# First product of the last stage by Strassen's scheme, with weight sums formed on chip and streamed from DRAM

## The chip, the cores and the metric

The program runs on one core of one Trainium2 chip. The metric is the device time of one execution in microseconds, read as the median of repeated executions; lower is better.

## What is computed

Attention with a decay mask on four batches of 576 positions, then a mixture of eight experts with two picks for each token, then an MLP whose activation is h cos h. All inputs are float32. Cut to what matters:

```python
x = attention(q, k, v).reshape(2304, 512)
for e in range(8):
    h = np.maximum(x[mask] @ w1[e], 0.0)
    out[mask] += top2_w[mask, k, None] * (h @ w2[e])
x = out                       # 2304 x 512
h = x @ w_in                  # 512 x 2048: the first product of the last stage
g = h * np.cos(h)
return g @ w_out              # 2048 x 512
```

## The kernel before

Every large product is made of three matmuls: each operand is split into a high part in fp32r, written by ScalarE (ACT), and the rest, written by VectorE (DVE), and high times high, low times high and high times low are summed in PSUM. A stationary tile is always 128x128; the moving tile has as many columns as there are tokens in the block (first products), or 512 columns of the output (second products).

**Attention** (lines 1216 to 1286) makes the tokens' rows and the gate's logits. GpSimd scatters each row into the slots of its two experts in DRAM (`x_slots`).

**Experts.** A unit is 640 slots of one expert, five tiles of 128. TensorE walks the units g in a loop; in a unit, step f (0 to 7) makes `product1(g, f + 1)` (line 1303, 24 matmuls of 320 columns), `product2(g, f)` (line 1321, 15 matmuls of 512), and, for f below 5, `transpose_x(g + 1, f)` (line 1209), which turns tile f of the next unit's rows and waits for its load `gath_in`. Meanwhile the weights of the next unit go through the buffer `raw` (two chunks of 512 KB): ACT writes `w_hi` (`w_high`, line 674), DVE `w_lo` (line 1038). SyncE (SP) issues nearly all transfers, in the order of its program and on one queue: in `unit_loads(g)`, for each f, the rows `gath[f]` (line 429) and the ring's chunk (`load_ring`, line 435); after them eight blocks of zeros into `y_slots` (line 446) in units 1 to 5, and the five `store_rows` of the unit's results (line 442). Each `gath[f]` is loaded in the same unit in which its tile is turned. Here unit 0 is written out, units 1 to 6 are the loop, and unit 7, the last, is written out apart (lines 1397 to 1442); during it ACT and DVE also split the sixteen chunks of the last stage's weights (`w_high_last`, `w_low_last`, lines 755 and 1054) into the buffers `w_hi`, `w_lo`, `w2_hi`, `w2_lo`, where all of them stay.

**Last stage.** Six blocks of 384 tokens (TB). `mlp_step(t, f)` on TensorE (line 1444) makes chunk f of 128 hidden features with 12 matmuls of 384 columns (line 1458), and, three steps later, its part of the second product with 9 matmuls of 512 columns (line 1477) into the PSUM banks 0 to 2. Between them a chunk goes ACT, DVE, DVE, ACT, ACT, DVE, ACT, DVE: `turns` (line 797), whole turns (1165), `angle` (1168), abs (802), sin (804), times h (1173), `g_hi` (809), `g_lo` (1176). GpSimd gathers the two expert rows of each token (line 586), ACT and DVE weigh and add them (731, 1109), TensorE turns them (1394), ACT and DVE split them (737, 1116). Outputs leave through ACT and DVE copies of the banks.

## Time and profile before

| | |
|---|---|
| median of 3 executions | 995.12 us (995.02 to 997.41) |
| the profiled execution | 993.64 us |
| its span | 991.7 us |
| TensorE (PE) busy | 973.3 us, 98% |
| weight loads (PEld) busy | 879.6 us |
| VectorE (DVE) busy | 486.5 us |
| ScalarE (ACT) busy | 425.3 us |
| GpSimd (POOL) busy | 104.1 us |
| moved by DMA | 122.02 MB |
| granted TensorE clock over the span | 0.998 |

A row of a group gives the line, the engine, the operation, what is written from what, the shape and the count, then the busy time, the mean duration of one, and the idle time before them with what ended it. Matmuls are pipelined: the duration of one is longer than the distance from one start to the next, and it is the distance that fills TensorE's time.

### The profile page before, as it was taken

To read this page: it belongs to the slowest core of one execution; us is meant where nothing else is said; L and a number is where in the kernel's file an instruction comes from. 1 tells how busy PE (TensorE), PEld (TensorE's weight loads), DVE (VectorE), ACT (ScalarE), POOL (GpSimd) and SP (SyncE) were. 2 spreads that over 40 slices of the span, in tenths; PEclk is the share of its full clock that TensorE was granted. 3 is DMA by queue.
4 is the path that set the end of the run, shared out by engine and by line. 5 is a ranking of instruction groups with operands and counts; after the bars stand their busy time and mean duration, and the time that the engine had idled before them with its cause. 6 is when DMAs were issued, how large, how long until landed. Compare 5 with 4: busy or idle time off the path is not lost.

```text
span 991.7 us, 17311 instructions
## 1 busy us (share of the span) xinstructions
PE 973.3 (98%) x6108; PEld 879.6 (89%) x6108; DVE 486.5 (49%) x944; ACT 425.3 (43%) x779; POOL 104.1 (10%) x106
## 2 busy tenths in 40 slices
PE   8999899999999999999999989999999999999997
PEld 7989789898989988898989979999999999999996
DVE  4788644333334333433434475555555555555554
ACT  1445334233233332332334465555455554545553
POOL 2276500000000000000000231000000001010000
PEclk9999999999999999999999999999999999999999
DMA  9988444436263542626315641010010101010000
GB/s 363 345 321 302 162 165 154 160 109 212 82 225 114 159 168 97 221 95 196 125 71 175 225 164 43 22 46 30 21 53 21 53 21 42 32 42 21 32 0 33
DMA packets 64359, 122.02 MB, mean 123 GB/s; under 512 B 5696, under 2 KB 31552, under 8 KB 64320
## 3 DMA queue, kind: packets, MB, share of 16 engines
q1 hardware_dynamic: 58080, 101.05, 29.7%
q0 software_dynamic: 6240, 20.45, 6.2%
q8 instruction: 25, 0.41, 0.2%
q14 instruction: 14, 0.11, 0.0%
HBM read 83.73 MB, written 37.75 MB: 122 GB/s over the span
## 4 chain that ended last, share of the span: by engine, by line
PE 86%; DMA 5%; issue 3%; POOL 2%; SPq 2%; DVE 1%; ACT 1%; ACTq 0%; POOLq 0%; DVEq 0%
PE ps L1458 20%; PE ps L1477 20%; PE ps L1303 15%; PE ps L1321 14%; PE ps L1209 2%; DMA gath<-x_slots 2%; PE ps L1339 2%; PE ps L1224 2%; PE ps L1407 2%; PE ps L1351 2%; PE ps L1247 2%; PE ps L1419 2%; DMA y_slots<-y_sb 1%; PE ps L1239 1%; POOL x_slots L540 1%
## 5 line engine op out<-in xcount | busy, mean ns | idle before, releaser
L1303 PE MATMUL ps<-xs,w_hi 128*128 (+1 forms) x784 | 182.9, 312 | 0.0
L1038 DVE TENSOR_TENSOR w_lo<-raw,w_hi 128x1024 fp32r<-128x1024 f32 x48 | 58.8, 1225 | 170.8 <-ACT w_hi L674 170.8
L1303 PEld LDWEIGHTS ps<-xs,w_hi 128*128 128x128 f32 x784 | 133.1, 188 | 0.8
L1458 PE MATMUL ps<-x_hi,w_hi 128*128 (+1 forms) x384 | 130.8, 341 | 0.1
L1458 PE MATMUL ps<-x_hi,w_lo 128*128 (+1 forms) x384 | 129.1, 336 | 0.0
L1458 PE MATMUL ps<-x_lo,w_hi 128*128 (+1 forms) x384 | 129.1, 336 | 0.0
L797 ACT ACTIVATE turns<-ps 128x384 f32<-128x384 f32 x96 | 47.2, 491 | 184.2 <-PE ps L1458 184.2
L1303 PE MATMUL ps<-xs,w_lo 128*128 (+1 forms) x392 | 121.2, 309 | 0.0
L1165 DVE TENSOR_SCALAR turns<-turns 128x384 f32<-128x384 f32 x96 | 37.3, 388 | 168.1 <-ACT turns L797 168.1
L1477 PE MATMUL ps<-w_hi,g_hi 128*128 128x512 f32 x288 | 112.6, 391 | 2.1 <-DVE g_lo L1176 2.1
L1477 PE MATMUL ps<-w_hi,g_lo 128*128 128x512 f32 x288 | 113.3, 393 | 0.0
L1477 PE MATMUL ps<-w_lo,g_hi 128*128 128x512 f32 x288 | 113.3, 393 | 0.0
L674 ACT ACTIVATE w_hi<-raw 128x1024 fp32r<-128x1024 f32 x48 | 50.8, 1059 | 141.3 <-PE ps L1321 107.8
L1321 PE MATMUL ps<-w_hi,hs_lo 128*128 128x512 f32 x245 | 96.2, 393 | 0.0
L1321 PE MATMUL ps<-w_lo,hs_hi 128*128 128x512 f32 x245 | 96.2, 393 | 0.0
L1321 PE MATMUL ps<-w_hi,hs_hi 128*128 128x512 f32 x245 | 95.8, 391 | 0.0
L668 ACT ACTIVATE hs_hi<-ps 128x320 fp32r<-128x320 f32 x98 | 42.3, 437 | 79.3 <-PE ps L1303 79.3
L1458 PEld LDWEIGHTS ps<-x_hi,w_hi 128*128 128x128 f32 x384 | 72.1, 188 | 3.7 <-issue 0.5
L1458 PEld LDWEIGHTS ps<-x_hi,w_lo 128*128 128x128 f32 x384 | 72.1, 188 | 3.1
L1303 PEld LDWEIGHTS ps<-xs,w_lo 128*128 128x128 f32 x392 | 73.7, 188 | 0.8
L1458 PEld LDWEIGHTS ps<-x_lo,w_hi 128*128 128x128 f32 x384 | 72.1, 188 | 0.0
L586 POOL DMA_INDIRECT y<-y_slots,pos_now x42 | 41.8, 995 | 276.3 <-PE ps L1394 266.9
(167 smaller groups left out, 1649.4 us busy)
## 6 DMA issues: line engine op xcount, KB each, us to landing
raw<-weights SPq DMA_DIRECT2D x80, 512.0 KB
y_slots<-zeros_sb SPq DMA_DIRECT2D x42, 256.0 KB, 3.6
gath<-x_slots SPq DMA_DIRECT2D x40, 256.0 KB, 3.5
y_slots<-y_sb SPq DMA_DIRECT2D x40, 256.0 KB, 2.1
qk<-qk SPq DMA_DIRECT2D x18, 512.0 KB
kv<-kv SPq DMA_DIRECT2D x18, 512.0 KB
out<-out_sb SPq DMA_DIRECT2D x18, 256.0 KB, 2.1
x_slots<-zeros_sb SPq DMA_DIRECT2D x8, 256.0 KB, 7.7
```

The source lines that it names most:

```text
L586: nc.gpsimd.indirect_dma_start(out=y[j][:, :], out_offset=None, in_=y_slots, in_offset=bass.IndirectOffsetOnAxis(ap=pos_now[:, k, j:j + 1] ...
L668: nc.scalar.activation(hs_hi[:, par, half * HALF:(half + 1) * HALF], ps[5 + half][:, 0:HALF], ACT.Relu).then_inc(relu_done, 1)
L674: nc.scalar.activation(w_hi[:, f * CHUNK:(f + 1) * CHUNK], raw[:, f % 2, :], ACT.Copy).then_inc(hi_done, 1)
L797: nc.scalar.activation(turns[f % 2][:, :], h_bank(f)[:, 0:TB], ACT.Copy, scale=PER_TURN, bias=ROUND).then_inc(turn_done, 1)
L1038: tt(w_lo[:, at], raw[:, f % 2, :], w_hi[:, at].bitcast(F32), ALU.subtract).then_inc(split_done, 1)
L1165: ts(whole[:, :], whole[:, :], -ROUND, None, ALU.add).then_inc(whole_done, 1)
L1209: last_one = nc.tensor.transpose(x_bank(g, j)[:, k * BLK:(k + 1) * BLK], gath[j][:, k * P:(k + 1) * P], ident)
L1224: last_one = nc.tensor.matmul(ps[half][0:C, n * C:(n + 1) * C], qk_sb[t % 3][rows, 1, n, :], qk_sb[t % 3][rows, 0, n, :], start=True, stop ...
L1303: last_one = nc.tensor.matmul(ps[5 + half][:, 0:HALF], w[:, at:at + P], xs[:, bass.ds(g % 2, 1), a, k, half * HALF:(half + 1) * HALF].rear ...
L1321: last_one = nc.tensor.matmul(ps[j][:, :], a[:, f % 2, j * BLK:(j + 1) * BLK], w[:, at:at + DM], start=f == 0 and i == 0, stop=f == FE - 1 ...
L1458: last_one = nc.tensor.matmul(h_bank(f)[:, 0:TB], w[:, cols], a[:, bass.ds(par, 1), k, :].rearrange("p a s -> p (a s)"), start=k == 0 and ...
L1477: last_one = nc.tensor.matmul(ps[j][:, :], a[f2 % 2][:, rows], w[:, cols], start=f2 == 0 and i == 0, stop=f2 == FT - 1 and i == 2)
```

## The change

**The scheme.** The hidden features are taken in eight pairs of chunks (`FP`), the tokens in four blocks of 384, 640, 640 and 640 (`SIZES`), each in two halves (`HALVES`: 192, 320, 320, 320). A slot is one block and one pair: 32 slots. In a slot the first product is a 2x2 block product (the two halves of the 512 input dimensions, the two chunks of the pair, the two halves of the tokens). It is made of seven products (`strassen(slot, o)`, 6 matmuls each of 192 or 320 columns) in place of eight. Both operands need sums: four of the weights (S), four of the tokens. Each of the seven results is copied or added into `p1_sb`, `u2`, `u3`, `u4` and the four quarters `h_sb` by ACT (one) and DVE (seven operations, `drain`). Only PSUM banks 5 and 6 hold these results (`p_bank`), so product i waits until product i - 2 has been taken away. The second product keeps its tile shape, as steps of 3 matmuls (`second`) for each tile and chunk, put between the seven products of the next slot. `h` is scaled to turns beforehand, through the gates (`gate1` times 1/2pi), which takes away one DVE operation of each chunk; the outputs are scaled back (`TURN`).

**The weights.** ACT and DVE form, for each pair, the high and low parts and the sums in `stage1` and `stage2`, in units 1 to 4 of the experts, two pairs in a unit (`pair_high`, `pair_low`). SP stores each pair into new DRAM tensors `w1_pairs` and `w2_pairs` and reads them back in every slot (`load_w1`, `load_w2`). A pair is 2 x 512 KB read, and 1.835 MB + 1.049 MB stored. The splitting in the last unit falls away. The six-block loop becomes straight code; block 0's tokens are split with the sums in `x_first`, the others in `x_odd` and `x_even`.

```diff
+SIZES = (3, 5, 5, 5)
+HALVES = tuple(n * C // 2 for n in SIZES)
+SLOTS = NBK * FP
+A11, A12, A22, S_FROM, A_W = 0, 256, 512, 768, 1792
+ORDER = ((A11, 0), (A12, 1), (S_FROM + 256, 4), (S_FROM + 512, 5), (A22, 6), (S_FROM, 3), (S_FROM + 768, 2))
+DRAINED = (0, 1, 2, 3, 4, 6, 7)
+PREP_UNITS = FP // 2
```

SP, the pairs' transfers and the streamed weights:

```diff
+            def load_pair(i):
+                if i >= 2:
+                    sp.wait_ge(pair_lo, 4 * (i - 1))
+                for half in range(2):
+                    sp.dma_start(raw_pair[i % 2][:, half, :], weights[E * FE + 2 * i + half]).then_inc(pair_in[i % 2], 16)
+            def store_pair(i):
+                sp.wait_ge(pair_lo, 4 * (i + 1))
+                sp.dma_start(w1_pairs[i].rearrange("p (a n) -> p a n", a=2), stage1[i % 2][:, :, :].bitcast(F32)
+                             ).then_inc(pair_out[i % 2], 16)
+                sp.dma_start(w2_pairs[i].rearrange("p (a n) -> p a n", a=2), stage2[i % 2][:, :, :].bitcast(F32)
+                             ).then_inc(pair_out[i % 2], 16)
+            for i in range(2):
+                load_pair(i)
             for j in range(TPU):
                 store_rows(0, j)
+            def next_pair(i):
+                store_pair(i)
+                if i + 2 < FP:
+                    load_pair(i + 2)
...
                     load_ring(g, f, e_next)
+                    if isinstance(g, int) and g <= PREP_UNITS and f == 4:
+                        next_pair(2 * (g - 1))
...
-            with sp.Fori(1, E - 2) as g:
+            for g in range(1, E - 2):
                 unit_loads(g)
                 for j in range(E):
                     zero_block(E * TPU + j + (g - 1) * E)
                 for j in range(TPU):
                     store_rows(g, j)
+                if g <= PREP_UNITS:
+                    next_pair(2 * (g - 1) + 1)
...
+            def load_w1(slot):
+                if slot >= 2:
+                    sp.wait_ge(p_done, 7 * (slot - 1))
+                sp.dma_start(w1_sb[slot % 2][:, :, :].bitcast(F32), w1_pairs[slot % FP].rearrange("p (a n) -> p a n", a=2)
+                             ).then_inc(w1_in[slot % 2], 16)
```

DVE, the low parts and the sums of the weights (ACT's `pair_high` writes the high parts of the same 1024, 512, 256 and 1024 columns); both stand in step f of unit g behind the splits of w and x:

```diff
+            def pair_low(i, q):
+                src = raw_pair[i % 2]
+                if q == 0:
+                    dve.wait_ge(pair_hi, 4 * i + 1)
+                    tt(stage2[i % 2][:, 1, :].rearrange("p (b n) -> p b n", b=2), src[:, :, DM:CHUNK],
...
+                if q == 2:
+                    a11, a12 = src[:, 0, 0:2 * P], src[:, 0, 2 * P:4 * P]
+                    a21, a22 = src[:, 1, 0:2 * P], src[:, 1, 2 * P:4 * P]
+                    link(tt(sums[:, 0, :], a21, a22, ALU.add))
+                    link(tt(sums[:, 1, :], sums[:, 0, :], a11, ALU.subtract))
+                    link(tt(sums[:, 2, :], a11, a21, ALU.subtract))
+                    tt(sums[:, 3, :], a12, sums[:, 1, :], ALU.subtract).then_inc(pair_sums, 1)
+                if q == 3:
+                    dve.wait_ge(pair_hi, 4 * i + 4)
+                    tt(stage1[i % 2][:, 1, S_FROM:A_W], sums[:, :, :].rearrange("p m n -> p (m n)"),
+                       stage1[i % 2][:, 0, S_FROM:A_W].bitcast(F32), ALU.subtract).then_inc(pair_lo, 1)
...
+                    if isinstance(g, int) and g <= PREP_UNITS:
+                        pair_low(2 * (g - 1) + f // 4, f % 4)
```

DVE, the middle of one slot of the last stage (`reduce`, `product` and `g_low` are its part of the cosine chain; ahead of these lines stand `reduce`, `g_low`, `product`, `drain` and `g_low` for the end of the slot before and for product 1):

```diff
+                reduce(slot, 0)
+                drain(slot, 2, u2, p1_sb)
+                product(slot, 0)
+                g_low(slot, 0)
+                dve.wait_ge(drained, 7 * slot + 2)
+                drain(slot, 3, u3, u2)
+                if p == 0 and b > 1:
+                    rows_out(b - 1, 1)
+                if b + 1 < NBK:
+                    ahead(b, p)
+                dve.wait_ge(drained, 7 * slot + 3)
+                drain(slot, 4, h_sb[1], u3, True)
+                reduce(slot, 1)
+                drain(slot, 5, u4, u2)
+                drain(slot, 5, h_sb[2], u3)
+                product(slot, 1)
+                reduce(slot, 2)
+                g_low(slot, 1)
+                dve.wait_ge(drained, 7 * slot + 5)
+                drain(slot, 6, h_sb[3], u4)
+                product(slot, 2)
...
 PE:
+            def strassen(slot, o):
+                b, i, n = slot // FP, 7 * slot + o, HALVES[slot // FP]
+                w, m = ORDER[o]
+                if o == 0:
+                    pe.wait_ge(w1_in[slot % 2], 16 * (slot // 2 + 1))
+                if slot % FP == 0:
+                    pe.wait_ge(x_lo_done, 7 * b + o + 1)
+                if i >= 2:
+                    before = (i - 2) % 7
+                    if before == 0:
+                        pe.wait_ge(p1_copied, (i - 2) // 7 + 1)
+                    else:
+                        pe.wait_ge(drained, 7 * ((i - 2) // 7) + DRAINED[before])
+                x = x_of(b)
+                for k in range(2):
+                    cols = slice(w + k * P, w + (k + 1) * P)
+                    for j, (hl, a) in enumerate(((0, 0), (1, 0), (0, 1))):
+                        last_one = nc.tensor.matmul(p_bank(i)[:, 0:n], w1_sb[slot % 2][:, hl, cols], x[:, a, m, k, :],
+                                                    start=k == 0 and j == 0, stop=k == 1 and j == 2)
+                last_one.then_inc(p_done, 1)
...
+            BEHIND = {10: (1, 1, 2, 1, 2, 2, 1), 6: (1, 1, 1, 1, 1, 1, 0)}
+            for slot in range(SLOTS):
+                b, p = slot // FP, slot % FP
+                todo = steps_of(slot - 1) if slot > 0 else []
+                at = 0
+                for o in range(7):
+                    strassen(slot, o)
+                    if todo:
+                        for step_ in todo[at:at + BEHIND[len(todo)][o]]:
+                            second(slot - 1, *step_)
+                        at += BEHIND[len(todo)][o]
```

Here `ahead(b, p)` prepares the next block during slot p of block b: for each tile ACT weighs, DVE adds and ACT copies it, and for each block seven highs on ACT, seven lows and four sums on DVE, each twice as wide as a half.

**SP at the end of an expert unit before** (`raw` and `gath` are the ring's chunk and the rows, an ISA row is a count for a wait), from the ring's last chunk on; the loop then turns back to `gath`:

```order
L435 ISA [waits split_done]
L435 DMA raw<-weights 128x1024
L446 ISA
L446 DMA y_slots<-zeros_sb 512x1x128
...
L442 ISA [waits y_act]
L442 DMA y_slots<-y_sb 128x512
```

The same place in the change, between the stores of unit 1 and the loads of unit 2 (`w_pairs` are the new DRAM tensors):

```order
L500 DMA y_slots<-zeros_sb 512x1x128 x8
L496 DMA y_slots<-y_sb 128x512 [waits y_act]
...
L531 DMA w_pairs<-stage_1 128x3584 [waits pair_lo]
L533 DMA w_pairs<-stage_1 128x2048
L527 DMA raw_pair<-weights 128x1024 [waits pair_lo]
L527 DMA raw_pair<-weights 128x1024
L547 TENSOR_LOAD meta
L547 ISA x2
L548 TENSOR_LOAD meta
L548 ISA x2
L483 ISA [waits tx_done]
L483 DMA gath<-x_slots 128x512
```

Four transfers now stand ahead of the first rows and the first ring chunk of the next unit, and SP waits for DVE's last low part of the pair before it issues any of them.

**ACT at the start of the last stage in the change**, between the experts' last result and the first copy out of a Strassen product (`p_sb` is `p1_sb`):

```order
L871 ACTIVATE y_sb<-ps 128x512 [waits y_out1]
L857 ACTIVATE x_first<-first_sums 128x384 [waits x_sums] x3
L857 ACTIVATE x_first<-raw 128x384 [waits xT_copied]
L900 ACTIVATE p_sb<-ps 128x192 [waits p_done]
L907 ACTIVATE turns<-h_sb 128x192 [waits drained]
```

Before, `turns` followed the copy to `y_sb` directly; four copies of tokens and the copy of product 0 now stand between them.

## Rows read from the trace of the kernel before

**Rows 1.** The page, part 1: busy time of each engine, share of the span, instructions.
```profile
PE 973.3 (98%) x6108; PEld 879.6 (89%) x6108; DVE 486.5 (49%) x944; ACT 425.3 (43%) x779; POOL 104.1 (10%) x106
```
**Rows 2.** Windows: stretch, engines' busy time, granted clock, DMA share, GB/s.
```profile
10.00:14.00 4.00, 3.40 (x64) 2.97 (x62) 3.03 (x6) 0.60 (x1) 2.00 (x2) 1.00 1.03 407
22.00:26.00 4.00, 4.00 (x69) 3.64 (x70) 2.66 (x7) 1.14 (x2) 0.80 (x1) 1.00 1.04 397
200.00:560.00 360.00, 357.81 (x2027) 323.80 (x2026) 134.28 (x192) 122.94 (x201) 0.92 (x2) 1.00 0.45 148
576.00:640.00 64.00, 62.52 (x324) 57.07 (x325) 39.23 (x73) 37.68 (x72) 14.39 (x15) 1.00 0.26 83
```
**Rows 3.** Timeline, TensorE, one step of the last stage: start us, us, engine, what.
```profile
762.68 0.33 PE L1458 MATMUL ps<-x_hi,w_hi 128*128 x1
764.79 0.39 PE L1477 MATMUL ps<-w_hi,g_hi 128*128 128x512 f32 x1
766.87 0.60 PE L1394 MATMUL ps<-table_sb,y 128*128 128x128 f32 x4
767.23 0.42 PE L1458 MATMUL ps<-x_hi,w_hi 128*128 x1
```
**Rows 4.** Timeline, first and last matmul of the last stage.
```profile
575.99 0.44 PE L1458 MATMUL ps<-x_hi,w_hi 128*128 128x384 f32 x1
...
986.60 0.39 PE L1477 MATMUL ps<-w_hi,g_lo 128*128 128x512 f32 x1
```
**Rows 5.** Timeline, TensorE, an expert step at a unit's start.
```profile
227.79 0.31 PE L1303 MATMUL ps<-xs,w_hi 128*128 x1
231.30 0.40 PE L1321 MATMUL ps<-w_hi,hs_hi 128*128 128x512 f32 x1
235.47 0.65 PE L1209 MATMUL ps<-table_sb,gath 128*128 128x128 f32 x4 [0.56 <-DMA gath<-x_slots]
```
**Rows 6.** Timeline, TensorE, attention: matmuls of 16 columns, back to back.
```profile
91.73 1.07 PE L1275 MATMUL ps<-wg,xT 128*128 128x16 f32 x8
92.65 0.64 PE L1280 MATMUL ps<-table_sb,xT 128*128 128x128 f32 x4
```
**Rows 7.** Groups of DVE and ACT instructions with their shapes: busy, mean ns, idle.
```profile
L1038 DVE TENSOR_TENSOR w_lo<-raw,w_hi 128x1024 fp32r<-128x1024 f32 x48 | 58.8, 1225 | 170.8 <-ACT w_hi L674 170.8
L1173 DVE TENSOR_TENSOR angle<-ps,angle 128x384 f32<-128x384 f32 x96 | 53.4, 557 | 7.8 <-ACT angle L804 0.5
L1124 DVE SCALAR_TENSOR_TENSOR hs_lo<-ps,hs_hi 128x256 fp32r<-128x256 f32 x7 | 2.9, 419 | 2.7 <-ACT hs_hi L746 2.7
...
L809 ACT ACTIVATE g_hi<-angle 128x384 fp32r<-128x384 f32 x96 | 48.8, 508 | 1.7 <-PE ps L1477 1.7
```
**Rows 8.** Waits: engine, line waited for, total us, times, longest.
```profile
PE ps L1209 <- DMA gath<-x_slots: 6.8, 7, 3.3
```
**Rows 9.** Timeline, SP's issues at the same unit's start.
```profile
226.14 4.07 SPq L442 DMA_DIRECT2D y_slots<-y_sb  x5
232.60 0.36 SPq L429 DMA_DIRECT2D gath<-x_slots  x1
```
**Rows 10.** Timeline, ACT and DVE at the same unit's start.
```profile
229.54 1.05 ACT L674 ACTIVATE w_hi<-raw 128x1024 fp32r<-128x1024 f32 x1
238.05 1.06 ACT L674 ACTIVATE w_hi<-raw 128x1024 fp32r<-128x1024 f32 x1 [6.11 <-DMA raw<-weights]
243.12 1.06 ACT L674 ACTIVATE w_hi<-raw 128x1024 fp32r<-128x1024 f32 x1 [2.88 <-PE ps L1321]
250.51 1.06 ACT L674 ACTIVATE w_hi<-raw 128x1024 fp32r<-128x1024 f32 x1 [3.00 <-PE ps L1321]
...
230.62 1.23 DVE L1038 TENSOR_TENSOR w_lo<-raw,w_hi 128x1024 fp32r<-128x1024 f32 x1 [1.66 <-ACT w_hi L674]
```
**Rows 11.** DMA issues: tensor, issuer, count, KB each, median us to landing.
```profile
y_slots<-y_sb SPq DMA_DIRECT2D x40, 256.0 KB, 2.1
...
wg<-gates_w SPq DMA_DIRECT2D x1, 32.0 KB, 7.7
```

More of the change, by code:

```diff
@@ L300, in logit_bank, with x2_bank @@
             return ps[7 - k % 2]
-        def walk_mlp(eng, step, tail=0):
-            for f in range(FT):
-                step(0, f)
-            with eng.Fori(1, NTB) as t:
-                for f in range(FT):
-                    step(t, f)
-            for f in range(tail):
-                step(NTB, f)
-        PREP_AT = (4, 8, 12)
-        def x2_bank(t, j):
-            return ps[j] if isinstance(t, int) and t == 0 else ps[3]
-        O_BANK = (2, 3)
+        def x2_bank(n):
+            return ps[n] if n < 3 else ps[{4: 3, 5: 4, 7: 3}.get(n, 7)]
@@ L321, in x_bank, with outs @@
+        def outs(b, j, odd_ones):
+            return sum((n + 1) // 2 if not odd_ones else n // 2 for n in SIZES[:b]) + j // 2 + 1
         def x_bank(g, j):
@@ L1185, in _, with drain @@
-            walk_mlp(dve, mlp_step, MLP_LAG + 1)
+            x2_sum(0, 2)
+            x2_sum(0, 3)
+            for at in range(2, 7):
+                x2_low(0, at)
+            def drain(slot, o, to, other, subtract=False):
+                n, i = HALVES[slot // FP], 7 * slot + o
+                dve.wait_ge(p_done, i + 1)
+                p = p_bank(i)[:, 0:n]
+                if subtract:
+                    tt(to[:, 0:n], other[:, 0:n], p, ALU.subtract).then_inc(drained, 1)
+                else:
+                    tt(to[:, 0:n], p, other[:, 0:n], ALU.add).then_inc(drained, 1)
@@ new lines, in g_low, with rows_out @@
+            def g_low(slot, q):
+                n, c = HALVES[slot // FP], 4 * slot + q
+                part, half = QUARTERS[q]
+                cols = slice(half * n, (half + 1) * n)
+                dve.wait_ge(g_hi_done, c + 1)
+                tt(g_lo[:, slot % 2, part, cols], angle[q][:, 0:n], g_hi[:, slot % 2, part, cols].bitcast(F32), ALU.subtract
+                   ).then_inc(g_split, 1)
+            def rows_out(b, j):
+                tile = FIRST_TILE[b] + j
+                dve.wait_ge(m2_done, final_step(b, j))
+                if b == 0 and j == 1:
+                    dve.wait_ge(y_all, 1)
+                above(dve, out_out[tile % 3], 16 * (tile // 3))
+                ts(out_sb[tile % 3][:, :], ps[j][:, :], TURN, None, ALU.mult).then_inc(out_dve, 1)
@@ L1486 @@
+            for step_ in steps_of(SLOTS - 1):
+                second(SLOTS - 1, *step_)
 def kernel(q, k, v, moe_w_gate, moe_w_noise, moe_noise, moe_w1, moe_w2, moe2_w_in, moe2_w_out):
```

676 lines of the change are left out of this document (422 added, 254 removed).

## The prediction

> **What bounds the kernel now.** I read the page first: TensorE is busy for 973.3 of 991.7 us and no other engine for half of that [rows 1]. So only two things can change the time: how long TensorE's instructions fill it, and new waits of TensorE. The windows say where it waits now: 2.2 us in the experts' 360 us, and 1.5 us in the first 64 us of the last stage [rows 2]. The clock is granted in full there, so every length below is one at 2.4 GHz. The timeline gives the true price of a matmul, the distance between starts. A step of the last stage is 2.11 us for 12 matmuls of 384 columns and 2.08 us for 9 of 512, and four transposes add 0.36 us [rows 3]. 96 steps and 15 transposed tiles make 402.2 + 5.4 = 407.6 us; from the first to the last matmul the stage takes 411.0 us [rows 4], so 3.4 us are waits at its ends. In the experts 24 matmuls of 320 columns take 3.51 us, 0.146 each [rows 5].
>
> The waits view has the row that matters most here: TensorE waits for the rows `gath` seven times, 6.8 us in all [rows 8]. Most of it is before unit 1, half a us at each later unit's start. It is small, but it says that the first load of each unit has no slack. In the timeline SP issues it at 232.60, and TensorE starts its transpose at 235.47, 2.87 us after, having waited [rows 5, 9].
>
> **The first product.** A slot of 320 columns fills TensorE for 42 x 0.146 + 30 x 0.231 = 6.13 + 6.93 = 13.06 us; 24 of them 313.4 us. For 192 columns no row exists. From 320 columns down, 0.029 us go with each 64 columns (0.146 at 320, 0.176 at 384), which gives 0.088 us. But eight matmuls of only 16 columns, each with its own 128x128 stationary tile, start 0.115 us apart (91.73 to 92.65) [rows 6]: there is a floor that columns don't lower. I take 0.112, by the row of 16 columns, since a Strassen matmul also changes its stationary tile each time; the ends are 0.088 and 0.115. A slot of 192 columns is then 42 x 0.112 + 18 x 0.231 = 4.70 + 4.16 = 8.86 us, eight of them 70.9 us. With the transposes the stage's filled time is 313.4 + 70.9 + 5.4 = 389.7 us against 407.6: **17.9 us less**. The seven-for-eight saving is there for 320 columns and is turned round for 192: 4.70 us where the same tokens cost 4.22 (two steps) before.
>
> The Trainium skill (TensorE: Matmul & The Clock Gate, "Back-to-back issue gap") gives a warm gap of N/2.4 + 2.5 ns, 82.5 ns for 192 columns; by it block 0 would cost 42 x 0.0825 x 8 = 27.7 us, an estimate, in place of 37.6. The 0.115 us between starts of 16-column matmuls disagree with that rule, and the row decides here; it stays as a rival.
>
> **New waits in the last stage.** DVE and ACT get more work and only two banks hold products. A DVE operation costs 0.419 us at 256 columns, 0.557 at 384, 1.225 at 1024 [rows 7]; between and beyond I take 0.35 at 192, 0.49 at 320, 0.82 at 640. A slot has 19 on DVE: 9.3 us of 13.06 at 320 columns, which fits, and 6.7 of 8.86 at 192.
> - Slot 0: product 2 waits for ACT's copy of product 0, which stands behind the last experts' copy and four copies of tokens (five of about 0.5 us by the 384-column row [rows 7]); the drains on DVE stand behind five low parts of 0.55 us. There is no second product to fill the gaps. I walk it to about 9.3 us for 4.7 of work, and slot 1 to 2 us late: +6.6.
> - Slots 6 and 7: DVE also makes one low and four sums, then five lows, 4.1 us each time, 10.8 us where TensorE needs 8.86: +1.9 twice, and about as much again since the two-bank hand-over leaves DVE no queue to work from. Slots 2 to 5: about +1 each with the tiles' adds. Block 0 in all: **+14**.
> - Opening block 1: the second product of tile 1 waits for DVE's copy of the old bank, which the program puts behind the drain of the next slot's product 1: +3.4.
> - The other slots of 320 columns: +0.2 each for late drains, +4. At the end the last chunk's chain, as before, 2.5.
>
> Together 24; the stage is 389.7 + 24 = 413.7 us against 411.0: **+2.7**. The gain is spent. With only slot 0 and DVE's bound it would be 10 (stage -11), with twice my waits 35 (+14).
>
> Weights: 2.88 MB a slot. Against a rate of 397 to 407 GB/s in the busiest windows [rows 2], 7.2 us of 8.86 in block 0 and of 13.06 later; with two gathered tensors for each tile (0.52 MB, 0.8 us a slot) block 0 just fits, and its slots are longer than that anyway. Cost 0; without that cover, rival B.
>
> **New waits in the experts: what decides.** ACT's added 3.1 us a pair (1024 + 512 + 256 + 1024 columns) and DVE's 5 us lie beside a TensorE that waits for neither. The transfers don't. At a unit's end SP now waits for the pair's last low part: ACT's `w_hi` ends at 230.6, its sums' high part at 231.6, DVE's `w_lo` ends at 231.85 and the low part 1.2 us later, 233.0 [rows 10]. Only then it issues a store of 1.835 MB, one of 1.049 MB, two loads of 0.52 MB, and behind them `gath[0]` and the ring's chunk, on one queue. That this queue is served in order shows in the transfers: 32 KB (`wg`) needed 7.7 us to land in the loaded first stage, 256 KB 2.1 us on an idle queue [rows 11]. At 390 GB/s, a little under the busiest windows since these are mostly stores, 3.93 MB are 10.1 us. `gath[0]` lands at 233.0 + 10.1 + 2.87 = 246.0 and TensorE, in order, stands at its transpose from 235.47: **10.5 us**, at the ends of units 1, 2 and 3. After unit 4 nothing is loaded: 2.88 MB, 7.4 us, 7.8 us late. Sum 39.3. The ring's chunk lands about 2 us after `gath[0]`, and what hangs on it has that slack.
> - The Trainium skill (DMA: Bandwidth & Descriptors, "Where 436 GB/s comes from") says that HBM transfers bind at about 358 GB/s; by it the four waits would be 3.4 us longer in sum, an estimate. The 407 GB/s of a window don't agree.
> - Inside a unit the even pair goes out in step 4, ahead of ring chunk 5. The steps are 7.39 us (243.12 to 250.51 [rows 10]); DVE is done with the pair 4.2 us into the step after 257.9, the backlog ends at 272.2 and the chunk lands near 276.5, wanted at 272.3. The late `w_hi`, and behind it two pair operations, hold back `relu` and `h_low` until about 1.1 us after TensorE wants them: 3 x 1.1 = 3.3 (ends 0 and 4 each).
> - Before unit 1 the first two pairs' loads (2.1 MB, 5.4 us) delay the y stores by about 2 us: 1.5.
>
> Experts: **+44.1**, ends 30 and 55. The last unit loses its splits, which TensorE didn't wait for: 0; its queue carries 6.8 MB (17.5 us) long before the y rows.
>
> **Sum.** 993.6 (the profiled execution) + 2.7 + 44.1 = 1040.4; the median of the runs is 1.5 us above that execution: **1042 us**.
>
> **Rivals.**
> A, faster: the transfers don't queue. If the sixteen rings serve the new transfers beside the old ones, `gath[0]` is only 1 us late at each of four units, the half-unit delay goes, and the stage decides: at its low end 995.1 + 4 + 1.5 - 11 = 989.6. It decides while a unit's wait stays under 1.5 us. Against it stand the 7.7 us of a 32 KB load, and that SP is held until 233.0, 0.4 us behind the old issue, in any case. Chance 0.09.
> B, slower still: the streamed weights or the stage's hand-overs bind. If reads with 2.88 MB a slot reach only 290 GB/s, a slot of block 0 is 11 us, +5, and with twice my stage waits +11: 1058; more with stores slower than 390 GB/s, up to 1070. For it: nothing in this trace stores so much. Chance 0.13.
> C, no floor under 192 columns: matmuls at 0.088 us, the lower end above, make 42 x 0.024 x 8 = 8 us less than my sum, 1034. DVE would bind block 0 at about the same length, so little of it would be seen. Chance 0.05. The Trainium skill's gap rule, named above, is this case.
> The forecast itself: 0.73.
>
> **Numbers.** About 0.3% (3 us) is what a measurement of this kernel tells from no change. A faster result needs A: 0.08; within 0.3% 0.02; slower 0.90. The range takes the experts' and the stage's low ends nearly together (995 + 30 - 7 = 1018) and reaches B's middle (1062); outside are A and B's tail.
>
> **What would show it.** In the changed profile: TensorE's wait for `gath<-x_slots` near 46 us in all with a longest of 10 to 11 us, four times at unit starts; SP's store of w_pairs issued some 3 us after the y stores; 42 matmuls of 320 columns in 6.1 us and of 192 in 4.7; block 0 about 85 us long, later slots 13.1 to 13.5. Right in sign for the wrong reason would be a stage far over 420 us with no long `gath` waits; wrong altogether if those waits stay under 2 us.

## The result, and the profile after

The changed kernel takes 1061.45 us (median of 4, 1058.85 to 1064.73) against 996.12 us for the kernel before on the same chip: 1.0657 times as long, interval 1.0623 to 1.0691. The forecast was 1042 us with 1018 to 1062.

| span of the profiled execution, by stretch | forecast | measured |
|---|---|---|
| up to TensorE's first transpose of unit 1 (176.77 before, 182.35 now) | +1.5 | +5.6 |
| waits for `gath` after units 1 to 4 | +39.3 | +45.2 |
| the rest of the experts (the last stage opens at 634.30, 575.99 before) | +3.3 | +7.5 |
| the last stage, first to last matmul (421.5 us, 411.0 before) | +2.7 | +10.5 |
| behind the last matmul | 0 | -1.4 |
| sum | +46.8 | +67.4 |

The second row is 13.09 + 12.53 + 13.12 + 8.25 less the same waits before, 0.56 [rows 5], 0.32, 0.48 and 0.46 us; the third is what is left of 58.3. The page, its row of engines, which answers to [rows 1], and the granted clock in tenths over 40 slices of the span:

```profile
PE 981.9 (93%) x6288; PEld 878.5 (83%) x6288; DVE 587.5 (55%) x1238; ACT 494.8 (47%) x976; POOL 96.6 (9%) x93
PEclk9999998997998998989999998999999999999999
```

TensorE is busy for 8.6 us more, in a span that is 67.4 us longer: what came is waiting. The waits view (waiter, line, what ended it, us in all, times, longest):

```profile
PE ps L1507 <- DMA gath<-x_slots: 54.2, 6, 13.1
PE ps L1757 <- ACT p_sb L900: 5.5, 10, 1.8
PE ps L1773 <- DVE out_sb L1408: 3.2, 1, 3.2
PE ps L1757 <- DVE h_sb L1378: 3.1, 2, 2.0
PE ps L1619 <- DVE y_sb L1228: 1.9, 1, 1.9
```

The first row answers to the 6.8 us of [rows 8]. The timeline shows one of these waits. SP's issues (start, length, what):

```profile
228.03 7.11 SPq L500 DMA_DIRECT2D y_slots<-zeros_sb  x8
235.25 5.28 SPq L496 DMA_DIRECT2D y_slots<-y_sb  x5
243.47 0.33 SPq L531 DMA_DIRECT2D w_pairs<-stage  x1
243.84 0.43 SPq L533 DMA_DIRECT2D w_pairs<-stage  x1
244.32 2.24 SPq L527 DMA_DIRECT2D raw_pair<-weights  x2
249.19 0.35 SPq L483 DMA_DIRECT2D gath<-x_slots  x1
```

TensorE in the same timeline, with its last matmul ahead of the wait:

```profile
242.69 0.39 PE L1619 MATMUL ps<-w_hi,hs_lo 128*128 128x512 f32 x1
256.17 1.11 PE L1507 MATMUL ps<-table_sb,gath 128*128 128x128 f32 x4 [13.09 <-DMA gath<-x_slots]
```

ACT there, a copy of y, a pair's high part and the first split of the next unit:

```profile
239.50 0.60 ACT L764 ACTIVATE y_sb<-ps 128x512 f32<-128x512 f32 x1 [4.09 <-DMA y_slots<-y_sb]
240.95 1.05 ACT L817 ACTIVATE stage<-sums 128x1024 fp32r<-128x1024 f32 x1
257.35 1.06 ACT L757 ACTIVATE w_hi<-raw 128x1024 fp32r<-128x1024 f32 x1 [14.70 <-DMA raw<-weights]
```

And DVE, a copy of y and the pair's last low part:

```profile
238.78 0.69 DVE L1228 COPY y_sb<-ps 128x512 f32<-128x512 f32 x1 [3.95 <-DMA y_slots<-y_sb]
242.23 1.22 DVE L1298 TENSOR_TENSOR stage<-sums,stage 128x1024 fp32r<-128x1024 f32 x1
```

From the store of the pair (243.47) to the transpose (256.17) it is 12.7 us; the forecast had 13.0. But the store itself is late. The copies of the y rows waited about 4 us for earlier y stores, 1.6 and 1.8 us before. Before, SP had issued the last store of zeros 1.8 us ahead of the first y store; now the ring's last chunks come late, behind the even pair's transfers, and the zeros end at 235.14, directly ahead of the y stores. So the pair's last low part ends at 243.4, when TensorE has just come to rest. The forecast had it 1.9 us ahead of TensorE.

The windows show what had not been in the forecast at all (stretch, busy times, granted clock, DMA share, GB/s):

```profile
243.00:260.00 17.00, 3.92 (x19) 3.84 (x19) 2.81 (x5) 2.52 (x4) 0.00 (x0) 0.60 0.88 339
460.00:475.00 15.00, 6.75 (x29) 6.25 (x29) 2.32 (x3) 1.98 (x3) 0.00 (x0) 0.66 0.87 319
636.00:650.00 14.00, 12.13 (x56) 11.43 (x57) 9.09 (x27) 8.22 (x23) 5.79 (x6) 0.63 0.69 236
745.00:850.00 105.00, 103.30 (x572) 91.44 (x572) 77.95 (x162) 69.87 (x146) 9.38 (x9) 1.00 0.58 223
```

In each long wait of TensorE and behind it, and in the first slots of the last stage, part of the stretch has the lower clock, 1.2 GHz in place of 2.4. Before, it was granted in full there [rows 2]. The four transposes behind the wait take 1.11 us, 0.65 before [rows 5].

The last stage by blocks (634.30 is its first matmul):

```profile
634.30:721.40 87.10, 79.47 (x483) 68.27 (x482) 60.85 (x167) 57.53 (x150) 15.62 (x16) 0.92 0.73 275
721.40:833.20 111.80, 107.43 (x585) 94.78 (x586) 80.04 (x169) 73.51 (x157) 10.24 (x10) 0.98 0.62 238
833.20:942.70 109.50, 107.80 (x597) 95.58 (x597) 81.83 (x170) 74.84 (x158) 4.09 (x4) 1.00 0.61 233
942.70:1055.80 113.10, 112.00 (x607) 99.52 (x606) 75.74 (x165) 70.22 (x151) 0.00 (x0) 1.00 0.52 196
```

Block 0 takes 87.1 us, about 85 in the forecast. In it the chain that ended last runs for long stretches between ACT and DVE alone, here in slot 4 (start, length, what):

```profile
676.55 0.46 ACT angle L915
677.03 0.37 DVE angle L1392
677.42 0.36 ACT g_hi L922
677.79 0.31 ACT angle L913
678.12 0.46 ACT angle L915
...
678.89 0.36 DVE h_sb L1380
679.27 0.37 ACT turns L907
```

### The profile page after: what moved, and what is told of

Read it like the earlier page. It is cut to its first block, busy times and chain, and to the rows that moved or that the text cites. A ratio compares the mean times of both kernels' runs of the same rounds, so it can differ in the third digit from the quotient of the medians.

```text
span 1059.1 us, 17609 instructions
## 1 busy us (share of the span) xinstructions
PE 981.9 (93%) x6288; PEld 878.5 (83%) x6288; DVE 587.5 (55%) x1238; ACT 494.8 (47%) x976; POOL 96.6 (9%) x93
## 4 chain that ended last, share of the span: by engine, by line
PE 59%; ACT 10%; DVE 10%; DMA 8%; SPq 5%; issue 5%; POOL 1%; DVEq 0%; ACTq 0%; POOLq 0%
PE ps L1601 11%; PE ps L1773 11%; PE ps L1619 10%; PE ps L1757 10%; DMA gath<-x_slots 3%; ACT angle L915 3%; DMA raw<-weights 3%; PE ps L1704 2%; ACT angle L913 2%; PE ps L1716 2%; DVE angle L1392 2%; SPq L500 2%; PE ps L1522 2%; DMA y_slots<-y_sb 2%; ACT g_hi L922 2%
## 5 line engine op out<-in xcount | busy, mean ns | idle before, releaser
L1773 PE MATMUL ps<-w_sb,g_hi 128*128 128x512 f32 x576 | 183.6, 400 | 3.2 <-DVE out_sb L1408 3.2
L1757 PE MATMUL ps<-x_odd,w_sb 128*128 128x320 f32 x672 | 118.2, 311 | 2.7 <-ACT p_sb L900 1.4
L1757 PEld LDWEIGHTS ps<-x_odd,w_sb 128*128 128x128 f32 x672 | 106.7, 189 | 14.8 <-issue 3.8
L1773 PE MATMUL ps<-w_sb,g_lo 128*128 128x512 f32 x288 | 113.2, 393 | 0.0
L1773 PEld LDWEIGHTS ps<-w_sb,g_hi 128*128 128x128 f32 x576 | 99.4, 191 | 10.5 <-issue 3.5
L907 ACT ACTIVATE turns<-h_sb 128x320 f32<-128x320 f32 (+1 forms) x128 | 56.4, 441 | 65.9 <-DVE h_sb L1378 55.3
L1392 DVE TENSOR_TENSOR angle<-h_sb,angle 128x320 f32<-128x320 f32 (+1 forms) x128 | 58.7, 458 | 47.9 <-ACT angle L915 45.7
L913 ACT ACTIVATE angle<-angle 128x320 f32<-128x320 f32 (+1 forms) x128 | 57.0, 445 | 36.2 <-DVE angle L1386 36.1
L1399 DVE TENSOR_TENSOR g_lo<-angle,g_hi 128x320 fp32r<-128x320 f32 (+1 forms) x128 | 58.5, 457 | 26.5 <-ACT g_hi L922 19.1
L922 ACT ACTIVATE g_hi<-angle 128x320 fp32r<-128x320 f32 (+1 forms) x128 | 57.0, 445 | 34.0 <-DVE angle L1392 31.5
## 6 DMA issues: line engine op xcount, KB each, us to landing
y_slots<-zeros_sb SPq DMA_DIRECT2D x42, 256.0 KB, 4.0
gath<-x_slots SPq DMA_DIRECT2D x40, 256.0 KB, 3.6
y_slots<-y_sb SPq DMA_DIRECT2D x40, 256.0 KB, 2.1
```

The lines of the kernel that those rows point to most:

```text
L907: nc.scalar.activation(turns[c % 2][:, 0:n], h_sb[q][:, 0:n], ACT.Copy, bias=ROUND).then_inc(turn_done, 1)
L913: nc.scalar.activation(a, a, ACT.Abs).then_inc(abs_done, 1)
L922: nc.scalar.activation(g_hi[:, slot % 2, part, half * n:(half + 1) * n], angle[q][:, 0:n], ACT.Copy).then_inc(g_hi_done, 1)
L1392: tt(angle[q][:, 0:n], h_sb[q][:, 0:n], angle[q][:, 0:n], ALU.mult).then_inc(g_done, 1)
L1399: tt(g_lo[:, slot % 2, part, cols], angle[q][:, 0:n], g_hi[:, slot % 2, part, cols].bitcast(F32), ALU.subtract).then_inc(g_split, 1)
L1757: last_one = nc.tensor.matmul(p_bank(i)[:, 0:n], w1_sb[slot % 2][:, hl, cols], x[:, a, m, k, :], start=k == 0 and j == 0, stop=k == 1 and ...
```

## Experiments on the experts' waits

Two questions: are these waits the place in SP's queue, and nothing of the change's own work on ACT and DVE? And what does the lower clock cost?

**r3_before_bulk**: the kernel before, with bytes alone (loads into a buffer that nothing reads, and SP's loop over the units written out).

```diff
                 for j in range(TPU):
                     store_rows(g, j)
+                for c in range(RING):
+                    sp.dma_start(bulk[:, c * CHUNK:(c + 1) * CHUNK], weights[c]).then_inc(bulk_in, 16)
...
```

> The kernel before, with eight loads of 0.52 MB (4.19 MB in all, into memory that nothing reads) issued by SP behind the y stores at the end of units 1 to 5, and nothing else of the change. Queue theory: SP issues them at about 230.3 on the clock of rows 9, they take 10.7 us at 390 GB/s, gath[0] lands 2.9 us behind them at 243.9, so TensorE waits 8.8 us at each of five unit starts, 44 us in all; the time is about 995 + 42 = 1037, or 1040 to 1045 if the clock is low after each wait. Rival (transfers share the rings, and the added work of ACT and DVE made the waits of the changed kernel): waits under 2 us, time under 1003.

Measured: 1045.60 us (two runs, 1044.21 and 1046.99), 1.0502 times before (1.0479 to 1.0526). SP's issues in its timeline:

```profile
231.80 4.27 SPq L493 DMA_DIRECT2D bulk<-weights  x8
237.49 0.35 SPq L432 DMA_DIRECT2D gath<-x_slots  x1
```

And its waits view:

```profile
PE ps L1215 <- DMA gath<-x_slots: 50.7, 8, 9.8
```

Eight loads of 0.52 MB between the y stores and `gath` make waits of 8.88, 9.79, 8.89, 8.79 and 8.90 us, with no sum of weights formed anywhere. So bulk transfers in that place of the queue are enough, without any work on ACT and DVE.

**r1_gath_ahead**: the odd pair's transfers behind the first `gath` of the next unit, and so in front of its first ring chunk.

```diff
                         load_rows(f, v_next)
+                        if f == 0 and isinstance(g, int) and 1 < g <= PREP_UNITS + 1:
+                            next_pair(2 * (g - 2) + 1)
...
-                if g <= PREP_UNITS:
-                    next_pair(2 * (g - 1) + 1)
```

> The changed kernel with gath[0] of units 2 to 5 issued ahead of the pair's stores and loads; ring chunk 0 stays behind them. Queue theory: TensorE's wait for gath falls from 54 us to under 10 in all, but chunk 0 lands about 14 us after the store is issued, ACT's w_hi holds back relu, and TensorE waits 8 to 10 us for DVE's hs_lo two products later; the time falls only to 1045 to 1055. Rival (the wait belongs to the rows alone, the ring has slack enough): no new wait, the time falls by about 45 to 1015.

Measured: 1051.64 us (two runs, 1049.76 and 1053.51). The wait moved to the next thing behind the transfers, as its waits view shows:

```profile
PE ps L1507 <- DVE xs L1200: 27.7, 4, 7.8
PE ps L1507 <- DMA gath<-x_slots: 11.7, 5, 4.5
```

The second transposes wait for DVE's low part of the tokens, which stands behind the low part of a weight chunk that came late; I had expected the wait two products later. Moving the bulk past one small load gives back 10 of 58 us, since the ring's chunk is as urgent.

**r2_warm**: matmuls of zeros in the waits, 52 after units 1 to 3 and 34 after unit 4 (TensorE's loop over these units is written out).

```diff
+                    if f == 0 and isinstance(g, int) and g > 1:
+                        pe.wait_ge(xs_done, TPU * (g + 1))
+                        for _ in range(52 if g < 5 else 52*2//3):
+                            nc.tensor.matmul(ps[7][:, 0:P], zeros_sb[:, :], zeros_sb[:, :], start=True, stop=True)
```

> The changed kernel with 52 matmuls of zeros (35 at the last) on TensorE ahead of its wait for gath[0] in units 2 to 5, into a bank that the transposes then overwrite; they fill the wait and take away none of it. Clock theory: the half clock that the profile shows from 2 to 3 us into each wait until 3 us behind it comes from the idle time; with it filled the granted clock stays full through these stretches, and the matmuls behind the wait run at full pace: 1.3 to 2 us less for each of four waits, 5 to 8 us in all, 1054. Rival (the clock falls for another reason, or costs nothing there): no change, 1061, or more if the zeros end later than the rows land.

Measured: 1058.08 us (1055.54 to 1061.15), 3.4 us less. Its window over the stretch that had 0.60:

```profile
243.00:260.00 17.00, 15.74 (x130) 15.33 (x129) 2.73 (x5) 2.23 (x6) 0.00 (x0) 1.00 0.89 339
```

The lower clock is gone there, and little comes of it: the two intervals against before overlap (1.0601 to 1.0658 and 1.0623 to 1.0691). It is a price of some 3 us, not of 10. The trace shows where some of the rest went: from the last matmul of a unit to the transposes it is now 48.0 us in sum for 47.0, and inside units 1 and 3 stand two waits of 0.83 and 0.92 us for DVE's `hs_lo` that the changed kernel does not have.

**r4_spread**: the same bytes in pieces, one or two behind each ring chunk (`behind_ring`); a pair's store is cut in three and its load in two, and the stores of zeros move to steps 0, 1, 4 and 5.

```diff
-                if g <= PREP_UNITS:
-                    next_pair(2 * (g - 1) + 1)
+                    if isinstance(g, int):
+                        behind_ring(g, f)
...
```

> The changed kernel with the same bytes moved in the experts, but each pair's store cut in three pieces and each load in two, one or two issued behind each ring chunk, and the zero blocks moved from the end of a unit to its steps 0, 1, 4 and 5. No step of 7.4 us then has over 2.4 MB (6 us). Queue theory: the gath wait falls to under 9 us in all, the half clock goes, and the experts take within 6 us of before; the time is about 1061 - 52 = 1008. Rival (the bytes or the added ACT and DVE work cost it, wherever they are issued): over 1035.

Measured: 1004.00 us (1001.53 to 1004.06). TensorE's waits for `gath` are 6.6 us in all, as before the change, and the last stage opens at 577.7. Nearly the whole of the experts' +58.3 us was the placement.

**p1_pool_queue**: the same transfers, whole, issued by GpSimd on its queue; SP's calls go.

```diff
+            for i in range(FP):
+                pool.wait_ge(pair_lo, 4 * (i + 1))
+                pool.dma_start(w1_pairs[i].rearrange("p (a n) -> p a n", a=2), stage1[i % 2][:, :, :].bitcast(F32)
+                               ).then_inc(pair_out[i % 2], 16)
+                pool.dma_start(w2_pairs[i].rearrange("p (a n) -> p a n", a=2), stage2[i % 2][:, :, :].bitcast(F32)
+                               ).then_inc(pair_out[i % 2], 16)
+                if i + 2 < FP:
+                    load_pair(i + 2)
...
```

> The changed kernel (1061.45 us) with only this moved: the loads and stores of the pairs (raw_pair<-weights, w_pairs<-stage) are issued by GpSimd, whose queue is empty then, instead of by SP. The same bytes at the same times, or a little earlier, since GpSimd waits for nothing but the pair's last low part. Theory (the waits are the order within SP's one queue, not the bytes): gath and the ring's chunks go beside the pairs' packets, TensorE's waits for gath fall from 54.2 us to 7 to 15 and the experts cost 2 to 12 us more than before the change: 1005 to 1016, best guess 1009. Rival (the 16 DMA engines are the limit and share alike, so that 256 KB beside 3.93 MB still land 5 us or more late): 1025 or more.

Measured: 1000.70 us (999.55 to 1001.34), 1.0057 times before (1.0042 to 1.0073); 61 us less than the changed kernel for one move of code, and better than my best guess of 1009. GpSimd's issues in its timeline:

```profile
234.37 0.54 POOL L659 DMA_DIRECT2D w_pairs<-stage  x1 [27.26 <-DVE stage L1290]
234.89 0.54 POOL L661 DMA_DIRECT2D w_pairs<-stage  x1
235.42 1.05 POOL L652 DMA_DIRECT2D raw_pair<-weights  x2
```

SP's first loads of the same unit start:

```profile
233.25 0.36 SPq L483 DMA_DIRECT2D gath<-x_slots  x1
233.88 0.35 SPq L489 DMA_DIRECT2D raw<-weights  x1
234.49 0.33 SPq L483 DMA_DIRECT2D gath<-x_slots  x1
```

TensorE's transpose:

```profile
236.03 0.65 PE L1499 MATMUL ps<-table_sb,gath 128*128 128x128 f32 x4
```

And the window that answers to the third of [rows 2]:

```profile
200.00:560.00 360.00, 360.00 (x2053) 327.52 (x2052) 157.08 (x241) 132.96 (x222) 17.72 (x31) 1.00 0.65 236
```

TensorE has no wait at the transposes at 236.03 with 3.9 MB on their way, and none in the 360 us in which it waited for 2.2 before [rows 2]. Two things changed with this one move, and the rows tell them apart. SP no longer waits for the pair's last low part, so the first rows leave 1.1 us ahead of GpSimd's first store, and the ring's first chunk 0.5 us ahead; at the other three unit ends the rows are 1.5 us ahead. The first rows land after 2.7 us (before, it was 2.87 us from their issue to the transpose [rows 5, 9]). The loads beside the bulk are slow: the second rows (234.49) take 8.2 us, the next chunk (235.08) 11.5 and the third rows (235.67) 12.9. The expectation's rival had this lateness (5 us or more), but TensorE wants the second rows only at 243.47, and they are there at 242.7. So the order of issue carries the first rows, and slack the later ones. No run has the whole bulk on SP's queue behind these first loads, so what the second queue adds to the order is not known.

The Trainium skill (DMA: Bandwidth & Descriptors, "Queues, rings and completion order") says that each DMA engine takes turns between the queues that have work. This run agrees: the second rows, issued 0.12 us behind the first store, land at 242.7, ahead of the pair's four transfers (243.5 to 252.1), where on the one queue the rows landed at 256.0, behind all four (249.2 to 255.4). The same page ("Issuing engines are not separate DMA queues") says that starting DMAs on several engines saves only the time to start them. That is too little here: starting these transfers takes SP 3.0 us a pair (0.33 + 0.43 + 2.24 above), some 20 us for eight pairs (the last two have no loads) and not on TensorE's path, and 61 us were saved, since the move also took a wait and the bulk's place in the order away from SP.

## Experiments on the last stage

With the experts repaired the kernel is still 5 to 9 us slower than before. These runs start from r4_spread.

**s2_no_stream**: is it the streamed weights?

```diff
-                if slot + 2 < SLOTS:
-                    load_w1(slot + 2)
-                    if slot >= 1:
-                        load_w2(slot + 2)
```

> The spread version (r4_spread, 1004.0 us) without the reads that stream the seven weight sums and the second product's weights in the last stage: the buffers are filled once and every later slot multiplies by what they hold, so the streamed reads (about 1.8 MB a slot and the second product's chunks) are left out. Theory (block 0 is held by the chain TensorE, VectorE, ScalarE at 192 columns, not by its supply): slots of block 0 stay at 10.0 to 10.7 us and the time within 3 us of 1004. Rival (the streamed reads come late in the short slots of block 0, as rival B of the prediction had it): the slots of block 0 fall towards 8.9 us and the time by about 10 us, to 994.

Measured: 1003.72 us (1001.28 to 1006.19). The kernel leaves out the reads and so multiplies by the wrong weights; the work of every engine is the same. Block 0 takes 87.2 us (86.9); its slots last 9.5 to 13.8 us as with the reads (10.0 to 12.8). Rival B's supply has no part in it.

**s3_stage_warm**: does the lower clock at the stage's start cost anything?

```diff
+                    if slot == 0 and o >= 2:
+                        for _ in range(7 if o == 2 else 2):
+                            nc.tensor.matmul(ps[7][:, 0:P], zeros_sb[:, :], zeros_sb[:, :], start=True, stop=True)
```

> The spread version with 19 matmuls of zeros more in slot 0 of the last stage (7 before its third product, 2 before each later one), into a PSUM tile that is still free. In r4_spread the granted clock is at its lower level for 10.2 us from 580.7, just behind the waits at the start of the stage. Theory (the lower clock there costs time): the stretch goes or shortens and the time falls by 2 to 4 us. Rival (TensorE waits for the sums of x there, so that the lower clock is hidden by the waits): no change, or up to 2 us more.

Measured: 1001.69 us (999.92 to 1002.27). Slot 0 went from 10.1 to 9.3 us, but the whole stage only from 421.3 to 420.7; the rest of the 2.3 us lies ahead of the edit, and the intervals overlap. Not settled, and small.

**s4_short_chain**: is it the chain of ACT and DVE? The kernel leaves out the turns, the whole turns and the abs of block 0, and its sine is a copy.

```diff
+                if slot < FP:
+                    act.sem_inc(abs_done, 1)
+                    nc.scalar.activation(a, h_sb[q][:, 0:n], ACT.Copy).then_inc(sin_done, 1)
+                    return
...
```

> The spread version without the range reduction of the cosine in block 0: its turns (ScalarE), the subtraction (VectorE) and the absolute value (ScalarE) are left out and the sine is a plain copy, so ScalarE does one pass for three on each of the 384-token hidden tiles of block 0 and VectorE one fewer. Theory (in block 0 the chain of VectorE and ScalarE per slot is longer than TensorE's 8.9 us): its slots fall from 10.0 to 10.7 us, and 12.6 to 12.8 for the last two, to about 8.9, and the time by 8 to 15 us, to 989 to 996. Rival (TensorE itself, or its weights' supply, sets 10.2 us a slot): slots and time stay within 3 us of r4_spread.

Measured: 993.21 us (989.51 to 1000.27, 10 runs), 10.8 us less. Block 0 takes 79.5 us instead of 86.9, its slots 9.3 to 10.7 and not the 8.9 expected. The stage's 7.3 us are the chain's (the stage of r4, r1, r2 and the changed kernel, all with the same last stage, takes 421.3 to 421.8 us); the other 3.5 lie ahead of the edit. Nothing was changed for TensorE or the transfers, so the chain holds block 0 for at least these 7 us; some 11 us above the filled time stay, and what they are is not shown.

**s5_both_warm**: only four of the seven high parts of block 0's tokens ahead of slot 0, the outputs of the block before leave PSUM first in their slot, and the zeros of s3.

```diff
+                if slot < SLOTS and p == 1 and b > 0:
+                    for j in range(1, SIZES[b - 1], 2):
+                        if j >= SIZES[b - 1] // 2:
+                            rows_out(b - 1, j)
...
+                if slot == 0:
+                    x2_low(0, 5)
+                    x2_low(0, 6)
```

> The best candidate: the spread version; in slot 0 of the last stage ScalarE and VectorE form only the first sums of x ahead and the rest behind the first drains; rows of the block before leave PSUM first in their slot instead of last (the 3.2 us wait of the second product at the second slot of block 1); and 19 matmuls of zeros in slot 0. Theory: first TensorE wait of the stage shorter by 1 to 2 us, the wait of 3.2 us gone, the clock's lower stretch at the start shorter: 996 to 1001, best guess 998. Rival (what is gained there is given back as waits of the next drains, since VectorE and ScalarE do the same work): 1001 to 1005. Neither expects it to beat the kernel before by 0.3%.

Measured: 997.50 us (994.88 to 999.09, 12 runs). Slot 0 takes 8.4 us for 10.1, the second slot of block 1 15.6 for 19.1, and the wait for `out_sb` is gone. The stage is 416.7 us.

**s6_pool_sums** and **s7_pool_sums_spread**: the token sums on GpSimd, and then the highs and lows in smaller groups.

```diff
-                        for i in range(4):
-                            x2_sum(1, i)
...
+                nc.gpsimd.tensor_tensor(t[:, i, :, :], first, second, ALU.subtract).then_inc(x_sums, 1)
```

> s5_both_warm (997.5 us) with the four sums of x of blocks 1 to 3 formed on GpSimd, which does nothing then, instead of on VectorE. In s5 those of block 1 stand on VectorE at 644.1 to 647.4 (815 to 826 ns each), between two drains, and TensorE's longest wait of the stage, with a step of 2.43 us between two matmuls at 647.74, ends with the drain behind them. GpSimd took 1271 ns for a product of 512 columns in s5, so about 1590 for 640 and 6.4 us for the four, in which nothing waits for them. Theory: that wait goes, 2 us less: 995.5. Rival (GpSimd beside VectorE slows VectorE's passes, or the sums come late for ScalarE): 997 or more.

> s6_pool_sums, and in the last slot of each block the highs and lows of the next block's x no longer stand together in front of one drain (in s5 five lows of 817 ns from 657.4 to 661.2, and a step of 1.42 us between matmuls at 661.51) but two or three at a time behind three of them. Theory: that wait of about 1 us goes too, and 0.3 us at the end of each later block: 1 to 2 us less than s6_pool_sums, 993.5 to 995, level with the kernel before (995.5) or at most 0.2% faster. Rival (the lows are then late for the first products of the next block): no change against s6_pool_sums.

Measured: 1003.95 us (1001.33 to 1007.47) and 1010.36 (1004.70 to 1012.64): both slower than s5 and not faster as expected, the second by 13 us. In the timeline of s6, GpSimd at the place in question:

```profile
648.71 2.24 POOL L725 TENSOR_TENSOR xT_sums<-xT_raw 128x640 f32<-128x640 f32 x1 [4.63 <-ACT xT_raw L890]
651.03 1.53 POOL L725 TENSOR_TENSOR xT_sums<-xT_raw,xT_sums 128x640 f32<-128x640 f32 x1
652.52 1.54 POOL L725 TENSOR_TENSOR xT_sums<-xT_raw 128x640 f32<-128x640 f32 x1
```

ACT, which comes to the next high part:

```profile
652.60 0.74 ACT L900 ACTIVATE x_odd<-xT_sums 128x640 fp32r<-128x640 f32 x1 [3.97 <-POOL xT_sums L725]
```

DVE, behind it:

```profile
653.62 0.66 DVE L1431 SCALAR_TENSOR_TENSOR angle<-turns,h_sb 128x192 f32<-128x192 f32 x1 [3.82 <-ACT turns L949]
654.20 0.34 DVE L1425 TENSOR_TENSOR u<-ps,u 128x192 f32<-128x192 f32 x1
```

I had overlooked that ACT's next high part needs the sums: it waits 3.97 us for GpSimd, and DVE behind it. And the 192-column pass of DVE beside a GpSimd pass takes 0.66 us, not 0.36; the next one, which reads PSUM, takes 0.34 beside GpSimd's fourth. A second loss stands in slot 1, ahead of any sum: DVE is idle for 2.91 us up to 591.05, and the trace gives no engine as the cause; with s7 the same, with s5 not, and the slot is 4 us longer than in s5 (13.8 for 9.7). I did not find out what it is. s7 leaves the waits for DVE's drains as they were (8.5 us, 9.2 in s6) and adds to those for ACT's copy of the first result (9.4, 4.9 in s6).

**p2_pool_stage**: the best of both halves, p1 with the stage of s5.

> p1_pool_queue with the edits of s5_both_warm in the last stage (order of the copies, 19 matmuls of zeros in slot 0), which were worth 6.5 us on r4_spread. Theory: 6 us less than p1_pool_queue; with p1 at its best guess 1003, at its low end 998. Rival (the two edits act on one thing, the late start of the stage): less than 3 us apart from p1. Neither expects it under the kernel before (996).

Measured: 994.76 us (993.10 to 996.36, 11 runs), 5.9 us less than p1 and 0.9997 times before (0.9988 to 1.0006). With everything repaired that I could, the change is worth nothing measurable: its stage takes 416.3 us against 411.0, and the experts 3.6 us less than before, of which 2.2 are waits for `gath` that the kernel before has in units 2 to 6 and this one has not.

## Why the prediction was right, and where it was short

The time lies inside the range, but only 0.6 us below its upper end, and 19 us above the forecast: all four terms came out too small, by 4.1, 5.9, 4.2 and 7.8 us. The mechanism was right; that the range held it is partly luck, since its end was rival B's middle, and only a part of B's causes came true.

- **The mechanism** ("that this queue is served in order") was right and carries the result. The pair's transfers between y stores and `gath` made the waits after the first four units. r3 makes such waits without the change; r1 sends the first rows ahead, and their waits fall to 1.2 to 1.9 us; r4 and p1 keep the bytes and lose the waits.
- **The term of the four waits**, 39.3, measured 45.2. The transfer time was right (12.7 us from store to transpose against 13.0), though 363 GB/s moved from 245 to 255 and not 390 (408 in r3, from 234 to 244, where the bulk is loads alone). The step that failed is "the low part 1.2 us later, 233.0": it took SP's time of issue from an undisturbed unit. The change delays the y stores, these the copies of y, and these the pair's last low part: about 2.3 us at the wait shown.
- **Before unit 1**, 1.5, measured 5.6: a wait of 1.86 us for a copy of y, and one of 4.09 for `gath` where there had been 1.37, both behind the first two pairs' loads.
- **Inside the units**, 3.3 (ends 0 and 4), measured 7.5, and by another cause. The step that failed is "hold back `relu` and `h_low`": the waits inside units 1 to 4 are one of 0.18 us. Units 1 to 4 last 2.6, 1.2, 1.2 and 2.4 us longer than before besides their waits, and they begin at the lower clock (0.50 in 182.4 to 187.4, 0.51 in 256.2 to 259.2, 0.50 in 328.1 to 330.8 and in 400.5 to 405.8), which the forecast never priced. r2 gives back only about 3 us of it, since the late chunks then show.
- **The first product** was right: from 767.29 on, groups of six matmuls of 320 columns fill 0.88 us, 0.147 each, and most later slots last 13.1 to 13.5 us (the last or first slot of a block 14.0 to 15.0, block 1's first two 11.6 and 19.1). For 192 columns the starts are 0.112 us apart (median), the value taken. So rival C is out: at 16 columns [rows 6] and at 192 the distance is nearly the same. The gap rule of the Trainium skill (TensorE: Matmul & The Clock Gate, "Back-to-back issue gap"), with its 82.5 ns, is out too; that section itself gives it for a matmul by itself and says that it counts too little at few columns, where the weight load is not in it. The forecast had overlooked a nearer row of the kernel before: at 256 columns (line 1339) the starts are 0.115 us apart.
- **Waits of the last stage**, 24, measured 31.8 (421.5 less 389.7). Opening block 1 was forecast at 3.4 and the wait is 3.2. The opening cost more than that wait, though: the slot lasts 19.1 us for 13.1 of filled time, and behind the wait the clock is at its lower level (0.50 in 740.5 to 743.7). Block 0 was +14 and is +18.5: its stretch has 68.6 us of filled time (70.9, less 4.2 of second products that slot 0 lacks, with 1.8 for five transposed tiles) and lasts 87.1. The term was computed from DVE's sum of work ("+1 each"); the chain shows that the hand-overs between ACT and DVE set these slots, though DVE is busy for 70% of the block and ACT for 66%, and s4 takes 7.3 us off.
- **A sum that is wrong**: the stage's high end, "with twice my waits 35 (+14)", is not twice 24. Twice 24 is 48, and the stage +27; rival B's 1058 would be 1071, and the range would have reached higher.
- **Rival A** (no queueing): r4 and p1 show what it would have been like, by another way. The waits are gone, and the kernel is still not faster, since p1's stage is at +12 us and not at the -11 that the rival took from its low end. **Rival B** reached the measured time and was half right: the stage's hand-overs did cost more than forecast (31.8 for 24, not twice), but s2 clears the streamed weights, and the stores were not slow enough to matter (12.7 us for 13.0).

The rows of the changed kernel's timeline for the first product at 320 columns:

```profile
767.29 1.04 PE L1757 MATMUL ps<-x_odd,w_sb 128*128 128x320 f32 x6
768.17 0.63 PE L1773 MATMUL ps<-w_sb,g_hi 128*128 128x512 f32 x2
```

## What to carry to other kernels

Before a bulk transfer is added, find the smallest load with no slack on the same issuing queue and see what stands between them; moving the bulk to a second queue cost one edit and was worth 61 us here, cutting and spreading it 57. Both put the first urgent loads ahead of it; loads beside the bulk took 8 to 13 us in the second queue too and need that much slack. One late transfer delays the work that releases the next, so take times of issue from the disturbed schedule. Fewer matmuls on TensorE pay only where the columns are wide and the engines that take up the results work as a pipeline: at 192 columns seven products cost more than eight at 384 had, and the chain of copies behind them cost more still.

## What the runs showed of the hardware that I had not expected

- Two queues share the DMA engines: 256 KB issued on SP's queue just behind the first of 3.9 MB on GpSimd's landed ahead of all of them (p1, at 242.7). It still took 8.2 us, where 256 KB issued 1.1 us ahead took 2.7.
- The granted clock fell to its lower level in each of TensorE's waits of 8 to 13 us and stayed there for 3 to 5 us behind them. It also fell in the first slot of the last stage, behind a wait of 1.8 us, where TensorE had been busy for 2.2 of 4 us (634 to 638): 0.50 in 638 to 648. With matmuls of zeros there it stayed at 1.00 (r2 in 243 to 260, s3 in 575 to 590).
- Beside GpSimd passes, two 192-column passes of DVE with both inputs in SBUF took 0.66 and 0.70 us instead of 0.36; two that read PSUM stayed at 0.34 (s6).
- A matmul with its own stationary tile starts 0.112 us after the last one at 192 columns and 0.115 at 16 [rows 6], and 0.115 at 256 (kernel before): under some 250 columns (0.112 on the line through 0.146 at 320 and 0.176 at 384, an estimate) narrower tiles buy no time.
